# First pair of token tiles computed as plain products in units of one tile, with its gate loaded tile by tile

## What is computed

```python
# 1. gated scan over the tokens
f = lower_bound + (1.0 - lower_bound) * sigmoid(f_logit)
h = f[:, t] * h + (1.0 - f[:, t]) * x[:, t]        # for t in range(S); y[:, t] = h
# 2. MLP, d_ff = 2048
g = leaky_relu(y @ w_in, 0.01);  z = g @ w_out
# 3. second MLP, its own weights
out = elu(z @ w_in2) @ w_out2
```

## Time and profile before

| | |
|---|---|
| median of 3 runs | 1047.2 us (1046.68 to 1047.95) |
| the profiled execution's own time | 1047.28 us |
| its span | 1045.5 us |
| mean granted TensorE clock | 0.991 of full speed |
| PE busy | 1018.5 us, 4360 matmuls |
| DVE / ACT / POOL busy | 881.9 / 616.0 / 55.7 us |
| moved by DMA | 40.32 MB |

### The profile page before, as it was taken

The page is one execution under the profiler, slowest core; times in us unless marked ns, Lnnn a source line. Parts: engine busy times, 40 slices in busy tenths (PEclk is TensorE's granted clock), DMA queues, the critical chain, the costliest instruction groups (busy, mean ns, idle before and its releaser), DMA issues.

```text
span 1045.5 us, 12492 instructions
## 1 busy us (share of the span) xinstructions
PE 1018.5 (97%) x4360; PEld 816.9 (78%) x4360; DVE 881.9 (84%) x1156; ACT 616.0 (59%) x945; POOL 55.7 (5%) x69
## 2 busy tenths in 40 slices
PE   6899999999999999999999999999999999999997
PEld 2677788888878878878888888888888888888886
DVE  6899788788888888878999888888888888888775
ACT  3545545544544553546676766666766666767564
POOL 3222000000000000002330000000000000000000
PEclk8899999999999999999999999999999999999999
DMA  3311300200210030012131020011011011001001
GB/s 105 131 41 41 119 0 1 89 33 1 68 54 1 1 120 1 1 58 82 41 91 51 1 75 4 1 41 41 1 41 41 1 40 41 1 1 41 1 1 40
DMA packets 20783, 40.32 MB, mean 39 GB/s; under 512 B 1776, under 2 KB 8944, under 8 KB 20720
## 3 DMA queue, kind: packets, MB, share of 16 engines
q1 hardware_dynamic: 20720, 39.53, 11.1%
HBM read 27.07 MB, written 12.45 MB: 38 GB/s over the span
## 4 chain that ended last, share of the span: by engine, by line
PE 90%; DVE 6%; issue 2%; DMA 1%; ACT 1%; POOL 0%; SPq 0%; DVEq 0%; ACTq 0%
PE y_ps L729 16%; PE y_ps L730 16%; PE y_ps L731 16%; PE a_ps L712 8%; PE a_ps L711 8%; PE a_ps L713 8%; PE c_ps L713 4%; PE c_ps L712 4%; PE c_ps L711 4%; PE b_ps L712 2%; PE b_ps L711 2%; PE b_ps L713 2%; DVE g_lo L579 1%; DVE w_in_lo L448 1%; DMA f_in<-f_logitT 1%
## 5 line engine op out<-in xcount | busy, mean ns | idle before, releaser
L729 PE MATMUL y_ps<-g_hi,w_out_hi 128*128 128x512 f32 (+1 forms) x768 | 303.7, 395 | 10.3 <-DVE g_lo L579 9.3
L731 PE MATMUL y_ps<-g_hi,w_out_lo 128*128 128x512 f32 (+1 forms) x768 | 301.6, 393 | 0.0
L730 PE MATMUL y_ps<-g_lo,w_out_hi 128*128 128x512 f32 (+1 forms) x768 | 301.6, 393 | 0.0
L729 PEld LDWEIGHTS y_ps<-g_hi,w_out_hi 128*128 128x128 f32 x768 | 144.5, 188 | 49.9 <-DVE g_lo L579 14.9
L359 ACT CAST g_hi<-e 128x1024 fp32r<-128x1024 f32 (+1 forms) x96 | 100.1, 1042 | 123.1 <-DVE e L560 121.1
L731 PEld LDWEIGHTS y_ps<-g_hi,w_out_lo 128*128 128x128 f32 x768 | 144.4, 188 | 32.9
L730 PEld LDWEIGHTS y_ps<-g_lo,w_out_hi 128*128 128x128 f32 x768 | 144.6, 188 | 32.2
L711 PE MATMUL a_ps<-x_hi,w_in_hi 128*128 128x512 f32 (+1 forms) x384 | 152.3, 397 | 10.5 <-DVE x_lo L509 6.8
L712 PE MATMUL a_ps<-x_lo,w_in_hi 128*128 128x512 f32 (+1 forms) x384 | 151.5, 395 | 0.0
L713 PE MATMUL a_ps<-x_hi,w_in_lo 128*128 128x512 f32 (+1 forms) x384 | 151.5, 395 | 0.0
L579 DVE TENSOR_TENSOR g_lo<-e,g_hi 128x1024 fp32r<-128x1024 f32 (+1 forms) x96 | 116.8, 1217 | 6.9 <-ACT g_hi L359 2.2
(11 more groups left out here) (61 smaller groups left out, 1412.9 us busy)
## 6 DMA issues: line engine op xcount, KB each, us to landing
f_in<-f_logitT SPq DMA_DIRECT2D x10, 512.0 KB, 5.2
x_in<-xT SPq DMA_DIRECT2D x10, 512.0 KB, 6.5
mid<-result SPq DMA_DIRECT2D x10, 512.0 KB, 3.5
x_in<-mid SPq DMA_DIRECT2D x5, 1024.0 KB, 5.0
outT<-result SPq DMA_DIRECT2D x10, 512.0 KB, 2.8
w_in_raw<-w_in SPq DMA_DIRECT2D x32, 128.0 KB, 2.3
w_out_raw<-w_out SPq DMA_DIRECT2D x16, 256.0 KB, 3.2
f_in<-f_logitT SPq DMA_DIRECT2D x2, 480.0 KB, 4.9
```

What stands on the lines that cost most here:

```text
L729: nc.tensor.matmul(out, w_out_hi[:, p, at], hi, start=(p == 0 and j == 0), stop=False)
L730: nc.tensor.matmul(out, w_out_hi[:, p, at], lo, start=False, stop=False)
L731: last = nc.tensor.matmul(out, w_out_lo[:, p, at], hi, start=False, stop=(p == H - 1 and j == 1))
```

## The change

Only the first pair in the first MLP is treated differently; the leaky steps are now 40 (rounds 1 to 5) instead of 48, and a step `s` belongs to round `s // 8 + 1`.

- **Units.** The first pair is computed as 16 units of one tile and one `p`, in the order of `unit(i)`: tile and `p` are (0,0), (0,1), (1,0), (0,2), (1,1), (0,3), (1,2) and so on to (0,7), (1,6), (1,7). A unit makes four plain block products (12 matmuls, `unit_up`) and their part of the second product (12 matmuls, `unit_down`). The operands are `A11`, `A12`, `A21`, `A22` and the token blocks of one tile, with no sums.
- **Gate tile by tile.** `load_first(n)` loads f and x in four pieces of one block and one tile; tanh, forget (now on ScalarE), input, scan and split follow piece by piece.
- **Weights twice.** `load_a(p)` loads the raw blocks into a ring of three in `c` (`a0` from ScalarE's queue), for the plain products. `load_w_in(p)` loads the same blocks again into `w_in_raw` for the sums, which are cut later, beside the units (`split_w_in`, 128x512), and the last two in steps 0 and 1.
- **The second pair** is prepared during units 3 to 15.
- `bound` is loaded from ScalarE's queue; 30 warm-up matmuls instead of 40.

```diff
+    LEAKY_STEPS = HALF - H
+    STEPS = 2 * HALF - H
+    UNITS = 2 * H
+    RING = 3
-    WARM = 40
+    WARM = 30
+    def unit(i):
+        if i == 0:
+            return 0, 0
+        if i == UNITS - 1:
+            return 1, H - 1
+        return (0, (i + 1) // 2) if i % 2 else (1, i // 2 - 1)
...
@@ SyncE
+            def load_a(p):
+                if p >= RING:
+                    sp.wait_ge(a_ready, p - RING + 1)
+                raw = c[:, p % RING, :].rearrange("p (b c) -> p b c", c=P)
...
-            load_scan(0)
+            for n in range(3):
+                load_first(n)
+            load_a(1)
+            load_first(3)
+            load_w_out(0)
+            load_a(2)
+            load_w_out(1)
+            load_scan(1)
             load_w_in(0)
-            load_w_out(0)
-            for i in range(1, H):
-                load_w_in(i)
+            for i in range(2, H):
+                if i + 1 < H:
+                    load_a(i + 1)
                 load_w_out(i)
-                if i == 1:
-                    load_scan(1)
-            for r in range(R):
+                if i > 2:
+                    load_w_in(i - 2)
+            load_w_in(H - 2)
+            load_w_in(H - 1)
+            for r in range(1, R):
...
@@ ScalarE
+            def unit_extra(i):
+                if i == 0:
+                    split_w_out(0)
+                    first_split(2)
+                elif i == 1:
+                    first_split(3)
+                    split_w_out(1)
+                    split_a(2)
+                elif i % 2 and (i + 3) // 2 < H:
+                    split_a((i + 3) // 2)
+                elif i % 2 == 0 and i // 2 + 1 < H:
+                    split_w_out(i // 2 + 1)
+                if i == 3:
+                    tanh(1, 0)
+                if i == 4:
+                    forget1(0)
+                    tanh(1, 1)
+                if i == 5:
+                    forget1(1)
+                if i >= UNITS - GROUPS:
+                    split_x(1, i - (UNITS - GROUPS) + 1)
+                if i >= 5 and i % 2:
+                    split_w_in((i - 5) // 2)
...
+            for i in range(UNITS):
+                unit_pre(i, 0)
+                unit_pre(i, 1)
+                if i != 1:
+                    unit_extra(i)
+                unit_split(i)
+                if i == 1:
+                    unit_extra(i)
             for s in range(STEPS):
                 step(s)
...
             def extra(s):
-                r, p = divmod(s, H)
-                if r == 0 and p + 1 < H:
-                    split_w_in(p + 1)
-                    split_w_out(p + 1)
+                r, p = pair_of(s)
+                if s < 2:
+                    split_w_in(H - 2 + s)
...
@@ VectorE
+            def unit_after(i):
+                if i == 0:
+                    split_w_out(0)
+                    scan(0, 1, 1)
+                    first_split(2)
+                if i == 1:
+                    first_split(3)
+                    save_carry(0)
+                    split_w_out(1)
+                    split_a(2)
+                if i in (5, 6):
+                    scan_input(1, i - 5)
+                if 7 <= i < 11:
+                    scan(1, (i - 7) % 2, (i - 7) // 2)
...
+                if i >= UNITS - GROUPS:
+                    split_x(1, i - (UNITS - GROUPS) + 1)
+                if i >= 5 and i % 2:
+                    split_w_in((i - 5) // 2)
...
+            for i in range(UNITS):
+                unit_leaky(i)
+                unit_extra(i)
+                unit_split(i)
+                unit_after(i)
...
@@ TensorE
+            for i in range(UNITS):
+                unit_up(i)
+                if i > 0:
+                    unit_down(i - 1, (0, 1))
             for s in range(STEPS):
                 step(s)
```

More of the change, by code:

```diff
@@ L56, in pair_tokens, with pair_of, units_through @@
         return slice(tokens(r, 0).start, tokens(r, 1).stop)
+    def pair_of(s):
+        return s // H + 1, s % H
     def in_mlp(s):
-        return s % HALF + 1
+        return s + 1 if s < LEAKY_STEPS else s - LEAKY_STEPS + 1
+    def unit(i):
[4 more added lines that the diff above has]
+        return (0, (i + 1) // 2) if i % 2 else (1, i // 2 - 1)
+    def units_through(t, p):
+        return [unit(i) for i in range(UNITS)].index((t, p)) + 1
     x_h = xT.rearrange("(k p) s -> p k s", p=P)
@@ L244, in w_sums @@
                 a21, a11, a12, a22 = (w_in_raw[:, n, :] for n in range(4))
-                s1, s2, s3, s4 = (w_in_raw[:, n, :] for n in range(4, 8))
+                s4, s1, s2, s3 = (w_in_raw[:, n, :] for n in range(4, 8))
                 po.wait_ge(w_in_loaded, 2 * DMA * (i + 1))
@@ new lines, in first_split, with forget1 @@
+            def first_split(n):
+                k, t = FIRST[n]
+                sc.wait_ge(scan_ready, n + 1)
+                nc.scalar.copy(first_operand(x_hi, k, t), first_tile(x_in, k, t)).then_inc(x0_hi_ready, 1)
+            def forget1(k):
+                sc.wait_ge(tanh_ready, k + 1)
+                f = both_tiles(f_in, 1, k)
+                nc.scalar.activation(f, f, ACT.Identity, bias=f_shift[:, k:k + 1], scale=f_scale[:, k:k + 1]
+                                     ).then_inc(forget1_ready, 1)
@@ L416, in step @@
                 extra(s)
[L417 removed]
+                if s < LEAKY_STEPS:
                     split_w(s)
@@ L425, in step @@
                     copy_sums(r, 0, 0)
[L427 to L432, removed]
+            def unit_extra(i):
[21 more added lines that the diff above has]
+                    split_w_in((i - 5) // 2)
+            nc.scalar.dma_start(bound[:, :], lower_bound).then_inc(bound_loaded, DMA)
+            raw = c[:, 0, :].rearrange("p (b c) -> p b c", c=P)
+            nc.scalar.dma_start(raw[:, 0:2, :], w_in1[:, 0, :].rearrange("p (b c) -> p b c", c=P)).then_inc(a0_loaded, DMA)
+            nc.scalar.dma_start(raw[:, 2, :], w_in1[:, 1, P:D]).then_inc(a0_loaded, DMA)
+            nc.scalar.dma_start(raw[:, 3, :], w_in1[:, 1, 0:P]).then_inc(a0_loaded, DMA)
+            first_gate(0)
+            first_gate(1)
+            split_a(0)
+            first_split(0)
+            first_gate(2)
+            first_split(1)
+            split_a(1)
+            first_gate(3)
+            for i in range(UNITS):
[6 more added lines that the diff above has]
+                    unit_extra(i)
             for s in range(STEPS):
```

355 lines of the change are left out of this document (253 added, 102 removed).

## The result

The changed kernel takes 1070.65 us (median of 4 runs, 1068.93 to 1072.25) against 1046.94 us: 1.0227 times, 95% interval 1.0215 to 1.024, 23.7 us slower. The forecast was 1068.8 us. The profiled execution took 1072.25 us, the longest of the four; its span is 1070.5 us.

The account below looks back on a forecast made before the run. TensorE, busy 97% of the span, bounds the kernel; at most 10 to 20 us could be won at the front. Losses of 7.1 + 12.9 + 1.5 = 21.5 us on 1047.28 gave 1068.8 us, range 1051 to 1076.

Parts of the forecast that it names:

- The two mechanisms: First-pair w_out loads held behind SyncE's weight-sum waits, 17.2 us; third pair's gate load late at the pair border, 12.9 us.
- The first product: Opening: TensorE's first real product at 10.9 us, 8.2 us sooner than before.
- The first units: TensorE idles 2.4 us before unit_down(0) and 2.5 us before up(2), together 4.9 us.
- The wait behind the second pair's load: w_out(2), queued behind pair 1's load, lands at 34.0 us and delays unit_down(2): 3.7 us idle.
- Four round trips: w_out(4) to w_out(7) wait behind weight-sum splits on SyncE: 14.8 us per two units, 17.2 us idle in all.
- The clock: Half-speed TensorE work after idle stretches, up to the second pair's first product: 2.9 us (zero to 5).
- Units 4 and 14: Small waits: 0.5 us for ScalarE's extra work ahead of hi(4), 0.7 us for two VectorE splits in unit 14.
- The mark: TensorE's first product of the second pair: at 121.9 us against 112.2 before, 7.1 us lost after 2.6 us allowance.
- The border: Between the first two pairs, pair 2's late gate load delays ScalarE's y copies: 12.9 us lost, plus 1.5 half speed.
- Unit waits hidden: Rival: the w_out waits in the units are hidden, the border wait is not: 1051.6 us, chance 0.07.
- Border hidden: Rival: the pair-border wait is hidden, the unit waits are not: 1054.4 us, chance 0.06.
- The faster rival: Rival: w_in_raw turns over quickly enough that SyncE never stands at w_in_ready; both terms go: 1037 us, chance 0.08.

Follow-up runs that it names:

- The early w_out(2): Changed kernel with w_in(0), a(3) and w_out(2) issued ahead of the second pair's load: 1061.72 us.
- The border run: Changed kernel with the third pair's load issued between the second loads of weights 6 and 7, no longer behind both: 1061.7 us.
- The reordered: Changed kernel with the second weight loads one place later in SyncE's list, so w_out(4) goes ahead of w_in(1) and so on: 1058.49 us.
- loosened run: Changed kernel, SyncE's list untouched: first-MLP weight loads wait only until GpSimd formed the previous sums, and GpSimd waits for VectorE's cut: 1047.26 us.
- the narrowed wait: The 1034.5 us version with ScalarE's first cast in step 0 waiting for 15 finished units instead of 16: 1034.64 us.
- the two runs that did it: Changed kernel with either the third pair's load between weights 6 and 7 (1061.7 us) or its ScalarE tanh passes behind step 1's casts and copies (1061.94 us).
- the fastest version: Changed kernel with four transfer edits together: loosened sum waits, w_out before second weight loads, w_out(2) before pair 1's load, third pair's load moved: 1034.53 us.
- 26 fillers: Changed kernel with 26 matmuls of unused result ahead of the first y_ps of pair 1: 1070.76 us.
- 42: Changed kernel with 42 matmuls of unused result ahead of the first y_ps of pair 1: 1069.02 us.

## Why the prediction was right, point by point

The two mechanisms were right, and experiments show both. That the total came within 2 us is in part luck: idle time was put too high, half-speed work too low, and one step of the sum was wrong. Positions are those of the one profiled execution.

- **The first product.** 10.9 forecast, 11.43 measured. The second piece (block 1 of the first tile) was ready for tanh only at 6.83 and through ScalarE's forget pass at 8.25; I had let its input step start at 7.6, when its x had landed.
- **The first units.** 4.9 us of idle time forecast; 2.1 and 0.4 measured. The clock was 0.73 in the stretch from 20 to 25 us, so part of what I had as idle was slow work.
- **The wait behind the second pair's load.** Right in mechanism, the term was mis-sized: 3.7 forecast, 6.7 measured. w_out(2) was cast at 36.09 and not at 34.0, issued at 29.37: 6.7 us of landing behind 2.1 MB. And "up(3) ends at 33.2" does not follow from the terms before it: 10.9 + 72 x 0.218 + 4.9 is 31.5, which makes this wait 5.4 us and the mark 123.6. TensorE reached that point at 32.1. The early w_out(2) shows the cause.
- **Four round trips.** 14.8 us a round forecast, 14.1 to 14.7 measured. I had 17.2 us of pure idle time; it was 12.3 us idle (3.79, 2.09, 1.91, 4.48) and the rest half speed: TensorE's clock was 0.92 from 58 to 102 us and 0.83 from 102 to 122. The round hardly depends on TensorE, so slow matmuls and waiting trade one for one. The border run shows it: there the four waits were 4.0, 1.2, 3.5 and 2.2 us, and the `y_ps` behind them still came 14.3, 14.3 and 14.6 us apart. The reordered and the loosened run show the cause.
- **The clock.** This term was mis-sized most. From the first product to the mark I had 81.1 us of work, 27.0 idle and 2.9 for half speed. It took 114.0 us with 21.5 idle, which leaves 11.4 for half speed. Units 4 and 14, for which 1.2 us are in the 27.0, show no wait.
- **The mark.** 121.9 forecast, 125.4 measured: 10.6 us lost there, not 7.1. 1.7 of the 3.5 is the wrong step above. The rest is no more than the 3 us by which the mark differs between executions of the same list.
- **The border.** From the mark to the first `y_ps` of pair 1 I had 21.7 us; it took 22.6. The second gate landed 5.7 us after its issue (5.6 forecast). Missing in the prediction was the 2.7 us wait of TensorE before A22 in step 0, from a cast that waits for the end of unit 15; the narrowed wait shows this cause. VectorE's split of weights 6 came 8.1 us behind the one of weights 5, where I had 7.2. The idle time was 9.0 us instead of 12.8: TensorE arrived later, since the 2.7 us and half-speed work stood ahead of it.
- **Sum.** By the two profiled executions 25.0 us were lost, 10.6 to the mark and 14.4 behind it; forecast 21.5 as 7.1 and 14.4. By the medians it is 23.7.
- **The rivals.** "Unit waits hidden" was 1051.6; the run that hid them all but for the sums took 1058.5. Its mark came at 112.0, 7.3 us behind 121.9 - 17.2: the wrong step above (1.7), the later w_out(2) (1.7) and the 3.9 us of waits that stayed. "Border hidden" was 1054.4; the two runs that did it took 1061.7 and 1061.9. They took back 6.8 and 6.1 of the 14.4 us behind the mark; the wait before A22, half-speed work and, in one of them, 2.0 us before `y_ps` stayed. The faster rival's condition, no standing at `w_in_ready`, is what the loosened run made true. It gave 1047.3 and not 1037, because w_out(2) and 4 us at the border were still there; with these cured too it gave 1034.5.
- **By the Trainium skill**, "DMA: Bandwidth & Descriptors", section "Anatomy of one DMA — SWDGE (gpsimd) path", the rounds would have cost 2.4 us less. The median landing after is 3.1 us for w_out's 256 KB, so the row of before was the better price; these loads are issued by SyncE, and no run here shows GpSimd's path.

Left open: how the 7.7 us of the earlier start, the 5.2 us of added matmuls and VectorE's lighter load share in the 12.4 us of the fastest version. No run took them apart.

## What to carry to other kernels

When a queue's list is rewritten, go through it with the question what each wait holds back behind it: here one wait for a staging buffer delayed loads that had nothing to do with that buffer. The two edits that brought most were to wait for the last reader of the bytes instead of the last step of the whole chain, and to place loads in the order in which they are needed. Count half-speed work with the idle time: here waits of 2 to 7 us left about half as much again in slow matmuls. Then ask on the consuming engine what stands behind the instruction that waits for the load, and before moving it, whether the gain is larger than the work that it pushes elsewhere.

## What the runs showed of the hardware

- Half of a load's size did not halve its landing. The gate pieces of 240 KB took 5.0 us in the median and the x pieces 5.3, where pieces of 480 KB had taken 4.9 and 6.0. The w_in pieces of 64 KB into the ring took 3.9 us, those of 128 KB 3.6, while 128 KB into `w_in_raw` took 2.3. These pieces were issued in groups, so size and place in the group are not told apart.
- A landing depends on what is ahead: w_out's 256 KB took 2.7 us at least and 6.7 us behind the second pair's 2 MB.
- The granted clock fell to 0.5 even when TensorE had been at full speed until 5.2 us before (26 fillers), and stayed at 1.0 over the same 9 us when they were filled (42).
